# A Trainium2 kernel of delta-rule attention and two feed-forward networks: Gram banks evicted one by one, transposes of the inverse in two parts, two masked products issued at other places

## The reference

```python
k_n = k / (norm(k) + 1e-6)
for t in range(768):
    y[t] = q[t] @ state
    state += beta[t] * outer(k_n[t], v[t] - k_n[t] @ state)      # per batch and head
x = y as (3072, 384)
h = x @ w_in                                                     # 384 -> 2048
g = where(h >= 1, h, where(h <= -1, 0, (h + 1)**2 / 4));  x = g @ w_out          # 2048 -> 384
xn = x / rms(x) * rms_g
out = (silu(xn @ w_gate) * (xn @ w_val)) @ w_out2                # 384 -> 1536 -> 384
```

## Time and profile before

| | us |
|---|---|
| median of three runs | 1051.35 |
| the profiled execution | 1049.63 |
| its span | 1047.8 |
| TensorE busy | 1029.5 (98% of the span) |
| VectorE busy | 540.9 (52%) |
| ScalarE busy | 470.5 (45%) |
| TensorE's granted clock, mean | 0.999 of full speed |

### The profile page before, as it was taken

The page is one execution under the profiler, slowest core; times in us unless marked ns, Lnnn a source line. Parts: engine busy times, 40 slices in busy tenths (PEclk is TensorE's granted clock), DMA queues, the critical chain, the costliest instruction groups (busy, mean ns, idle before and its releaser), DMA issues.

```text
span 1047.8 us, 25033 instructions
## 1 busy us (share of the span) xinstructions
PE 1029.5 (98%) x11128; PEld 851.2 (81%) x11128; DVE 540.9 (52%) x1012; ACT 470.5 (45%) x845; POOL 9.5 (1%) x19
## 2 busy tenths in 40 slices
PE   8899899999999999999999999999999999999998
PEld 4599798777777777777788888888888888888886
DVE  6878469568647837843366444334234234333222
ACT  6755744754664574464476453232232232232221
POOL 1000000000000000000000000000000000000000
PEclk9999999999999999999999999999999999999999
DMA  9406005002300500120111220200200100100101
GB/s 265 133 13 142 3 4 139 14 3 62 92 3 32 122 3 3 52 102 3 61 61 61 82 100 1 61 1 1 61 1 19 43 1 1 31 1 1 31 1 30
DMA packets 19035, 48.10 MB, mean 46 GB/s; under 512 B 2448, under 2 KB 9232, under 8 KB 17872
## 3 DMA queue, kind: packets, MB, share of 16 engines
q1 hardware_dynamic: 18480, 45.72, 15.7%
q10 hardware_dynamic: 448, 0.79, 0.2%
HBM read 37.06 MB, written 9.44 MB: 44 GB/s over the span
## 4 chain that ended last, share of the span: by engine, by line
PE 90%; DVE 5%; ACT 3%; issue 2%; POOL 0%; ACTq 0%; POOLq 0%; DVEq 0%
PE bank L759 21%; PE hps L1337 19%; PE acc L1352 18%; PE acc L787 10%; PE hps L759 7%; PE hps L787 4%; DVE outer L1080 1%; DVE inv L1084 1%; PE bank L1296 1%; PE bank L1229 1%; PE bank L1282 1%; PE bank L1275 1%; PE bank L1258 1%; PE bank L1309 1%; PE bank L1217 1%
## 5 line engine op out<-in xcount | busy, mean ns | idle before, releaser
L667 ACT ACTIVATE g<-bank 128x512 f32<-128x512 f32 x72 | 43.1, 599 | 242.1 <-PE bank L759 129.1
L1337 PE MATMUL hps<-xh,w1h 128*128 128x512 f32 (+1 forms) x336 | 129.1, 384 | 3.7 <-DVE g L1165 2.3
L1352 PE MATMUL acc<-g1h,w2h 128*128 128x512 f32 (+1 forms) x336 | 126.8, 378 | 0.3 <-ACT x2s L1007 0.3
L1337 PE MATMUL hps<-xl,w1h 128*128 128x512 f32 (+1 forms) x336 | 122.2, 364 | 0.0
L1352 PE MATMUL acc<-g1l,w2h 128*128 128x512 f32 (+1 forms) x336 | 122.1, 364 | 0.0
L1337 PE MATMUL hps<-xh,w1l 128*128 128x512 f32 (+1 forms) x336 | 121.8, 363 | 0.0
L1352 PE MATMUL acc<-g1h,w2l 128*128 128x512 f32 (+1 forms) x336 | 121.8, 362 | 0.0
L999 ACT ACTIVATE g1h<-g 128x512 fp32r<-128x512 f32 (+1 forms) x112 | 63.9, 571 | 128.2 <-DVE g L1165 116.4
L1173 DVE TENSOR_TENSOR g1l<-g,g1h 128x512 fp32r<-128x512 f32 (+1 forms) x112 | 68.5, 612 | 91.1 <-ACT g1h L999 90.7
L1165 DVE SCALAR_TENSOR_TENSOR g<-hps,g 128x512 f32<-128x512 f32 (+1 forms) x112 | 68.1, 608 | 58.1 <-ACT g L993 58.1
L990 ACT ACTIVATE g<-hps,half_c 128x512 f32<-128x512 f32 (+1 forms) x112 | 69.7, 623 | 43.6 <-PE hps L1337 42.9
(11 more groups left out here) (218 smaller groups left out, 2034.6 us busy)
## 6 DMA issues: line engine op xcount, KB each, us to landing
kqT<-kq SPq DMA_DIRECT2D x22, 384.0 KB, 6.5
v_in<-v SPq DMA_DIRECT2D x6, 768.0 KB, 4.3
k_in<-k SPq DMA_DIRECT2D x6, 768.0 KB, 5.5
x2d<-x2s SPq DMA_DIRECT2D x18, 256.0 KB, 5.6
x2t<-x2d SPq DMA_DIRECT2D x6, 768.0 KB, 5.9
y<-y_t SPq DMA_DIRECT2D x44, 96.0 KB, 2.2
stage<-w_in SPq DMA_DIRECT2D x4, 768.0 KB, 8.8
stage<-w_gate SPq DMA_DIRECT2D x3, 768.0 KB, 4.3
```

The costliest lines, as they stand in the source:

```text
L667: act.activation(silu[:, f % 2, :], gps[f % 2][:, :], ACT.Silu).then_inc(e_silu, 1)
L1337: last = pe.matmul(hps[f % 2][:, 0:WIDTH[n]], wt[:, kk, P * f:P * f + P], xx[:, kk, COLS[n]], start=(kk == 0 and e == 0), stop=(kk == KD - ...
L1352: last = pe.matmul(acc[j][:, 0:WIDTH[n]], wt[:, f, P * j:P * j + P], gg[:, f % 2, 0:WIDTH[n]], start=(f == 0 and e == 0), stop=(f == NF1 - ...
```

## The change

Four edits. (1) In `inversion(c)`, for c >= 1, `ft` and `xd` become two units each, of 16 of the 32 rows, and each is placed by itself; the semaphore is raised by the second part. Their weights are 10 each, before 20 and 21. (2) The transposes of lines 1092 and 1095 take that part. (3) ScalarE's eviction of a Gram: before, the full copies of both banks, then the two corner copies of each; now copy and corners of the first bank, then those of the second. The corner copies wait for the full copy of their bank, as before. Only GK units of steps 2 to 5 (two per step) have two banks on ScalarE. (4) GQ(1,0) and GQ(1,1) are no longer in the list `us` ahead of KS, but are placed at `done + 54` and `done + 64` on the scale of 192.

By the formulas of `next_body` the new places are: GQ(1,0) right ahead of h(0.10), between o(0.7) and h(0.10), behind g(0.9) on VectorE; GQ(1,1) behind the first of the three units of o(0.9), and on VectorE between inv 17 and g(0.11). Both are in tile 0. `us` of body 1 loses two entries, and the units from X(1,0) to the end of the body stand one or two units of the network further apart. Around the transposes of body 1 VectorE's order becomes ft, g(1.1), ft, gl(1.1), xd, g(1.2), gl(1.2), xd, vn, g(1.3); before it was ft, g(1.1), gl(1.1), xd, g(1.2), gl(1.2), g(1.3), vn. In body 2 it becomes g(2.4), inv 30, ft, gl(2.4), ft, xd, g(2.5), xd, gl(2.5), vn, g(2.6); before inv 30, ft, g(2.4), gl(2.4), xd, g(2.5), gl(2.5), vn, g(2.6).

```diff
 def inversion(c):
...
-    return out + [(("ft", c, 0), 20), (("xd", c, 0), 21), (("vn", c, 0), 17)]
+    parts = range(2 if c else 1)
+    out += [((kind, c, n), 41 // (2 * len(parts))) for kind in ("ft", "xd") for n in parts]
+    return out + [(("vn", c, 0), 17)]
...
-        if e == ("xd", k, 0):
+        if e == ("xd", k, 1):
             turned = at
...
     if k == 1:
-        us.insert(us.index(("KS", k, 0)), ("GQ", k, 0))
-        us.insert(us.index(("KS", k, 1)), ("GQ", k, 1))
+        ev += [((done + 54 + 10 * hf) / total, ("GQ", k, hf)) for hf in range(HALVES)]
...
+            def turned_part(c, q):
+                return slice(BLK // 2 * q, BLK // 2 * q + BLK // 2) if c else slice(0, BLK)
...
                                act.activation(gram[c % 2][:, H * q:H * q + H, :],
                                               bank_of(u, j)[:, :].rearrange("p (i t) -> p i t", t=C), ACT.Copy).then_inc(s_gf, 1)
-                            for j in range(own):
-                                q = NQH * hf + j
                                 act.wait_ge(s_gf, done + j + 1)
                                 for r in UPPER:
...
-                            dve.transpose(tt[:, :, BLK:C].rearrange("p i t -> p t i"), inv[:, :, :]).then_inc(s_ft, 1)
+                            t = turned_part(c, q)
+                            last = dve.transpose(tt[:, :, BLK + t.start:BLK + t.stop].rearrange("p i t -> p t i"), inv[:, t, :])
+                            if t.stop == BLK:
+                                last.then_inc(s_ft, 1)
...
-                            dve.transpose(xd[:, :, :].rearrange("p i c -> p c i"), inv[:, :, :].rearrange("p t c -> p c t"))\
-                                .then_inc(s_ft, 1)
+                            t = turned_part(c, q)
+                            last = dve.transpose(xd[:, :, t].rearrange("p i c -> p c i"), inv[:, :, t].rearrange("p t c -> p c t"))
+                            if t.stop == BLK:
+                                last.then_inc(s_ft, 1)
```

## The result

| | before | changed |
|---|---|---|
| median, us | 1050.99 (6 runs) | 1057.07 (6 runs, 1055.37 to 1057.72) |
| profiled execution / its span | 1049.63 / 1047.8 | 1055.37 / 1053.6 |
| TensorE busy | 1029.5 | 1029.7 |
| mean granted clock | 0.999 | 0.996 |

What follows compares the result with a forecast made beforehand. TensorE, busy for 98% of the span, was taken as the bound. +8.0 at h(1.5), -0.95 crowded part, -2.6 for two GQs, -0.9 body 2 and 1.6 clock gave +5.15, so 1056.5 us, range 1053.0 to 1060.0.

Steps and rivals of the forecast that it cites:

- The load: At the moved GQ(1,0) in tile 0: queries land at 89.9, so TensorE stands from 82.4 to 90.0 us, 7.6 us.
- The clock: Behind the load's wait: a fall to 1.2 GHz costs between 0 and 3.3 us; the middle, 1.6 us, was taken.
- the rival with three blocks: Behind the load's wait: the clock falls and stays down for all three blocks, 1058.2 us; chance 0.26.
- the clock holds: Behind the load's wait: the clock stays at 1.00, 1054.9 us; chance 0.2.
- Up to h(1.5): From the load's wait to h(1.5): it starts at 118.35 instead of 110.35, 8.0 us late, without the clock term.
- The new wait behind xd and vn: Ahead of g(1.3) in body 1: xd and vn stand together, 2.7 us, and give 1.1 of the halves' gain back.
- The crowded part: Tile 1, where TensorE waits for ScalarE's evictions: 0.95 us gained, bounds 0 and 2.5, besides 2.6 for two GQs gone.
- Body 2: At h(2.6) and the second Gram: waits of 0.58 and 0.34 go, 0.9 us gained.
- The sum: Whole kernel: +3.55 us, with the clock +5.15, giving 1054.8 profiled and 1056.5 as median.
- The rival on the other side: At the moved GQ(1,0): the load is in time, no wait or clock fall, 3.0 us faster, 1048.3; chance 0.07.

Runs made afterwards that it cites:

- e1: The kernel before with edit (4) alone, GQ(1,0) and GQ(1,1) moved into tile 0; 1057.93 us, ratio 1.0062.
- e3: The changed kernel with SyncE issuing the queries of step 1 ahead of the load of v, some 40 us sooner; 1048.05 us, ratio 0.9981.
- e7: The changed kernel with the queries of step 1 loaded ahead of v once PU(0,0) is done, about 52 us; 1047.47 us, ratio 0.9961.
- e8: The changed kernel, loads unchanged, with GQ(1,0) and GQ(1,1) placed later, at done + 78 and done + 88; 1047.89 us, ratio 0.9966.
- e4: The changed kernel with seven added unit-matrix matmuls ahead of the wait for the queries, keeping TensorE busy; 1054.91 us, ratio 1.0047.
- e9: e7 with vn one unit later, so that it stands behind g(1.3) again; 1045.68 us, ratio 0.9947 to the kernel before.
- e5: The kernel before with edit (3) alone, each Gram bank copied and cornered before the next; 1051.05 us, ratio 0.9998.
- e11: e10 with edit (3) undone, both full copies of a Gram before the corner copies; 1045.36 us, ratio 0.9942 to the kernel before.
- e10: e9 with the copies of up(1,0) and up(1,1) on VectorE instead of ScalarE, four units later; 1045.30 us, ratio 0.9948 to the kernel before.
- e12: The kernel before with edit (4) and the load of e7, without edits (1) to (3); 1048.81 us, ratio 0.9984.
- e2: The changed kernel with edit (4) undone, GQ back in tile 1; 1050.28 us, ratio 0.9991 to the kernel before.
- e6: The kernel before with edits (1) and (2) alone, ft and xd in two parts, placed apart; 1050.11 us, ratio 0.9989.

## Why the prediction was right

**The load.** Landing forecast at 89.9, measured 89.86; the wait 7.6 against 7.12 us (TensorE comes 0.35 later in this execution, from before body 1: 76.33 against 75.98 at XT). It came from the time between issue and landing of the fourth DMA and from SyncE's order. e1, e3, e7 and e8 show that it is the cause: taken away by an earlier load or a later product, it takes the loss with it. The mechanism is right, but that the landing agrees to 0.04 us is luck: the same load landed at 91.4 in e1 and at 91.2 in e4.

**The clock.** The middle of 0 and 3.3, 1.6, was put in. Measured: GQ(1,0) +0.83 (89.99 to 91.91 against 1.09) and the block behind it +0.91 (91.91 to 93.91), 1.74 us. The Trainium skill ("TensorE: Matmul & The Clock Gate", Part 1 on the HAM clock gate) states that the array is throttled by default and that activity releases the throttle; the trace agrees: the engine came back at a granted clock of 0.50. In this trace the rival with three blocks was 1.6 us too high, but in e1's, with the same load, all three ran at 0.50 and the price was 5.92 - 3.27 = 2.65 us. So a fall was to be expected and its size varies between executions; that the middle fits is luck.

One reading under this term was wrong. The prediction takes from the earlier trace rows that the matmuls behind the idle 1.61 us ran at the full clock. The column of the granted clock says 1.00 there, but the durations don't: the four in that row fill 1.61 to 5.21 us, 0.90 each, and eight of the same shape a little later fill 7.45 to 10.99, 0.44 each:

```profile
7.45 3.70 PE L1363 MATMUL acc<-ident 128*128 128x512 f32 x8
```

In e4 the same shape takes 0.44 too. So the row shows half the pace at the start of the program. It doesn't say that a pause of 1.61 us brought it, and it was no ground for a lower end of 0 nor for the chance of 0.2 that the clock holds.

**Up to h(1.5).** Forecast 8.0 + 1.6 = 9.6 late; measured 119.77 - 110.35 = 9.42, of which 0.35 was there before. The new wait behind xd and vn was 1.15 in the working (118.35 against 117.2) and is 0.90. e9, where vn stands behind g(1.3) again, takes it away: 1.8 us less than e7 by the medians, 1.5 by the ratios, whose intervals overlap. That is more than the wait itself. The profile of e7 also had the half clock and that of e9 had not, which may be the rest; it isn't shown.

**The crowded part** is the mis-sized term. From h(1.5) to the first block of body 2 TensorE won back 9.42 - (167.24 - 160.36) = 2.54 us. The two GQs that no longer stand there are 2.6, so the gain of 0.95 from the waits is zero, its lower bound. GK(2,1), KS(1,0), U(1,0) and Z/X wait 1.0 + 0.6 + 0.9 + 0.7 = 3.2 us here; before, GK(2,1), GQ(1,0), U and Z/X waited 3.35. The prediction let KS wait 0.9 and U not at all; U waits for the subtraction on VectorE instead. e5 shows the same for the bank order.

**Body 2.** Forecast -0.9; measured from its first block to the end (1053.6 - 1047.8) - 6.88 = -1.1; neither wait of the earlier trace rows is left.

**The sum** in these terms is 9.42 - 2.54 - 1.08 = +5.8 between the two profiled spans, of which 0.35 was there before body 1, against +5.15. It came out close because two errors partly cancel: h(1.5) was 0.5 us less late than forecast by the changed part alone, and the crowded part gave 1.0 us less. The medians differ by 6.1.

**The rival on the other side** priced the kernel with the load in time at 1048.3; e3 and e7 gave 1048.05 and 1047.47.

## What to carry to other kernels

Before a product is moved forward in a static order, look up when its operand lands, not only whether its banks and engines are free: the row of the DMA, issue plus time to landing, against the time at which the engine comes to the new place. A wait in an engine that is otherwise full cost its length here and then 1.7 to 2.7 us of slow clock behind it. And where several units wait one behind the other, look at the sum of their waits and at the time, not at one wait: a bank freed sooner (e5, e11) and less work on the engine that evicts (e10) moved or shortened single waits by 0.2 to 0.6 us, and the time stayed. An agreement of the total with a forecast should be taken apart term by term as well; two of the hits here were luck.

## What the runs showed of the hardware

The half clock doesn't need a pause of 7 us. In five profiles it came behind TensorE's wait at GK(2,1) in tile 1, for some 3 us: e1 (wait of 1.80 us), e3 (1.52), e7 (1.48), e8 (1.49) and e12 (1.83). In the nine others the clock kept 1.00 behind waits at the same place: the kernel before (1.23, then 1.31 at GQ), the changed kernel (1.02), e2 (1.44, then 1.59), e4 (1.50), e5 (0.63, then 1.62), e6 (1.79, then 1.28), e9 (0.97), e10 (0.78) and e11 (1.11). So the length of the wait alone doesn't decide. e6 and e12 side by side (TensorE's timeline at GK(2,1), then length, busy, instructions, clock of the stretches from 120 to 130 us):

```profile
122.21 1.20 PE L1228 MATMUL bank<-kqT 48*64 48x64 f32 x64 [1.79 <-ACT gram L937]
...
120.00:125.00 5.00, 2.88 (x77) 1.00 0.01 3
125.00:130.00 5.00, 4.05 (x142) 1.00 0.01 3
```
```profile
125.15 1.32 PE L1216 MATMUL bank<-kqT 48*64 48x64 f32 x64 [1.83 <-ACT gram L930]
...
120.00:125.00 5.00, 3.32 (x81) 1.00 0.00 0
125.00:130.00 5.00, 4.85 (x116) 0.68 0.01 3
```

What decides between them these runs don't settle. Nor are such falls seen in changed kernels alone: of the 23 executions of the kernel before beside e1 to e4, two had a mean clock of 0.994 and took 1054.2 and 1055.0 us, where most had 0.998 or 0.999 and a median of 1050.9. Where the clock fell in these two no trace tells.

How long TensorE works at half clock behind the same kind of wait varies too: it was back at some 93.7 us in the changed kernel, 3.7 us after the work began again, and at some 97.5 us in e1, 5.9 us after. The landing of the same DMA, issued within 0.2 us of the same time, varied by 1.6 us between traces (89.9 to 91.4).
